# Retention attention and two expert layers on one core: one causal mask for all steps, loads in another order, sums moved forward, paired transposes

## The reference

```python
for t in range(S):                       # q, k, v: (4, 8, 768, 64)
    state = gamma * state + k[:, :, t]^T v[:, :, t]
    y[:, :, t] = scale * q[:, :, t] @ state
x = y as (3072, 512)
h = x @ w_in                             # 512 x 2048
x = where(h > 0, h, exp(min(h, 0)) - 1) @ w_out
h = x @ w_in2                            # 512 x 1024
sm = exp(h - max) / (sum + 1e-9);  s = h * sm
out = ((s - mean(s)) / sqrt(var(s) + 1e-6) * g_ln) @ w_out2
```

## Time and profile before

| | us |
|---|---|
| median of 3 runs (lowest to highest) | 857.64 (855.99 to 858.91) |
| the profiled execution, as timed | 856.04 |
| its span | 854.3 |
| PE busy / DVE / ACT / POOL | 840.5 / 553.7 / 419.0 / 390.1 |
| attention stage, to the first product of the first expert stage | 86.3 |
| first expert stage | 86.3 to about 580 |
| second expert stage and its output | about 580 to 854 |

### The profile page before, as it was taken

How to read it: one execution, slowest core, us unless ns; L and a number is a source line. 1 busy time by engine, 2 the same in 40 slices (tenths; PEclk the granted TensorE clock), 3 DMA queues, 4 the chain that set the end, 5 groups by cost and what they waited for, 6 DMA issues and landing times.

```text
span 854.3 us, 12592 instructions
## 1 busy us (share of the span) xinstructions
PE 840.5 (98%) x4852; PEld 694.9 (81%) x4852; DVE 553.7 (65%) x848; ACT 419.0 (49%) x679; POOL 390.1 (46%) x446
## 2 busy tenths in 40 slices
PE   9997999999999999999999999999999999999998
PEld 6987788888888888888888888887878888888886
DVE  3585667677735455576345655788887777777773
ACT  4566665655525555544355565563333333333322
POOL 3577667575006657540256651464253343444200
PEclk9999999999999999999999999999999999999999
DMA  8999611013103001050111101613011111111001
GB/s 305 362 369 347 228 30 45 25 50 128 49 1 96 28 25 49 26 173 1 43 56 31 44 26 44 203 50 98 26 50 50 49 49 39 51 50 50 25 13 50
DMA packets 49359, 73.32 MB, mean 86 GB/s; under 512 B 3218, under 2 KB 23954, under 8 KB 49044
## 3 DMA queue, kind: packets, MB, share of 16 engines
q1 hardware_dynamic: 48864, 72.43, 25.2%
q10 hardware_dynamic: 436, 0.08, 0.0%
HBM read 55.73 MB, written 16.78 MB: 85 GB/s over the span
## 4 chain that ended last, share of the span: by engine, by line
PE 92%; DVE 4%; ACT 1%; issue 1%; POOL 1%; DVEq 0%; ACTq 0%; POOLq 0%
PE ps L673 10%; PE ps L677 10%; PE ps L674 10%; PE ps L626 9%; PE ps L628 9%; PE ps L627 9%; PE ps L783 5%; PE ps L785 5%; PE ps L784 5%; PE ps L685 4%; PE ps L687 4%; PE ps L686 4%; PE ps L576 3%; PE ps L603 3%; PE ps L769 2%; PE ps L589 1%
## 5 line engine op out<-in xcount | busy, mean ns | idle before, releaser
L494 POOL TENSOR_TENSOR u_lo<-u_raw,u_hi 128x256 fp32r<-128x256 f32 x168 | 142.0, 878 | 193.5 <-ACT u_hi L1117 193.5
L673 PE MATMUL ps<-g_hi,wd_hi 128*128 128x512 f32 x384 | 149.4, 389 | 0.0
L674 PE MATMUL ps<-g_hi,wd_lo 128*128 128x512 f32 x384 | 149.4, 389 | 0.0
L677 PE MATMUL ps<-g_lo,wd_hi 128*128 128x512 f32 x384 | 149.4, 389 | 0.0
L626 PE MATMUL ps<-x_hi,u_hi 128*128 128x512 f32 x336 | 131.3, 391 | 1.2 <-DVE u L888 1.2
L627 PE MATMUL ps<-x_hi,u_lo 128*128 128x512 f32 x336 | 130.8, 389 | 0.0
L628 PE MATMUL ps<-x_lo,u_hi 128*128 128x512 f32 x336 | 130.7, 389 | 0.0
L489 POOL TENSOR_TENSOR u_raw<-u_raw 128x256 f32<-128x256 f32 x96 | 88.7, 923 | 17.3 <-DMA u_raw<-w_dram 11.1
L677 PEld LDWEIGHTS ps<-g_lo,wd_hi 128*128 128x128 f32 x384 | 72.1, 188 | 15.0
L674 PEld LDWEIGHTS ps<-g_hi,wd_lo 128*128 128x128 f32 x384 | 72.1, 188 | 15.0
L673 PEld LDWEIGHTS ps<-g_hi,wd_hi 128*128 128x128 f32 x384 | 72.1, 188 | 14.9
(11 more groups left out here) (91 smaller groups left out, 1498.1 us busy)
## 6 DMA issues: line engine op xcount, KB each, us to landing
u_raw<-w_dram SPq DMA_DIRECT2D x24, 512.0 KB, 3.5
k<-units_dram SPq DMA_DIRECT2D x12, 512.0 KB, 6.4
q<-units_dram SPq DMA_DIRECT2D x12, 512.0 KB, 4.8
v<-units_dram SPq DMA_DIRECT2D x12, 512.0 KB, 7.3
x_between<-x SPq DMA_DIRECT2D x24, 256.0 KB, 2.7
x_raw<-x_between SPq DMA_DIRECT2D x12, 512.0 KB, 3.5
out_dram<-y_sb SPq DMA_DIRECT2D x24, 256.0 KB, 2.0
kn<-units_dram SPq DMA_DIRECT2D x10, 512.0 KB, 6.1
```

What stands on the lines that cost most here:

```text
L494: nc.gpsimd.tensor_tensor(u_lo[n % 2][:, o, :], u_raw[n % 2][:, o, :], u_hi[n % 2][:, o, :].bitcast(f32), ALU.subtract).then_inc(ul_done, 1)
L673: nc.tensor.matmul(ps[:, bank + m, :], hi, g_hi[:, no % 3, :], start=(f == 0), stop=False)
L674: nc.tensor.matmul(ps[:, bank + m, :], lo, g_hi[:, no % 3, :], start=False, stop=False)
L677: last = nc.tensor.matmul(ps[:, bank + m, :], hi, g_lo[:, no % 3, :], start=False, stop=(f == NF1 - 1))
```

## The change

It has five parts.

1. The table `mask0`, the two-row table and the three `spread_row` products go. A full-size `q_decay` table (256 KB) is loaded by SP first; DVE scales q of step 0, and POOL scales q of every later step, step 6 among them. All steps use the same causal mask. PE's warm-up products go from 6 to 13.
2. `load_step(s)` issues q(s), v(s), k(s) and natural k(s), all of the same step.
3. In the first expert stage, unit 0 does U3 ahead of the activation and the weight split, and unit 1's U2 is done ahead of the last activation of unit 0.
4. In the second expert stage DVE's sums for products 1 and 2 are done earlier, the moments being cut in two (`solu_spread`, `solu_variance`); in the last pair the second maximum is taken after the first tile's variance.
5. From the third pair on (`separate` is false) P7 comes before P5, P5 and P3 use bank 4 in place of bank 6, and both tiles of a pair are transposed one after the other, the odd one into banks 6 and 7.

```diff
-WARM = 6
+WARM = 13
...
+        def separate(u):
+            return u < 3
+        def P5(u):
+            return 4 if separate(u) else 5
+        def P7(u):
+            return 5 if separate(u) else 4
+        def w_bank(u):
+            return 6 if separate(u) else 4
+        def normed_bank(t):
+            return 0 if t < 4 else 6 * (t % 2)
...
-                step_over(s - SLOTS)
-                load(s, v_sb, 3, v_in)
-                if s + 1 < NS:
-                    step_over(s + 1 - SLOTS)
-                    load(s + 1, q_sb, 0, q_in)
+                if s >= SLOTS:
+                    sp.wait_ge(att_done, s - SLOTS + 1)
+                load(s, q_sb, 0, q_in)
+                load(s, v_sb, 3, v_in)
+                load(s, k_sb, 1, k_in)
                 if s % NC < NC - 1:
                     load(s, kn_sb, 2, kn_in)
-                if s + 1 < NS:
-                    load(s + 1, k_sb, 1, k_in)
...
-            load(0, k_sb, 1, k_in)
-            load(0, q_sb, 0, q_in)
+            sp.dma_start(q_decay[:, :], tables[:, T_QDEC:T_QDEC + HH * C]).then_inc(q_decay_in, 16)
...
-                if (s + 1) % NC > 0:
+                if s + 1 < NS:
                     decay_q(s + 1)
...
-                if u > 0:
-                    pe.wait_ge(h2_summed, sums(u - 1, H12))
-                up_product(u, W, S1, T1, True)
+                if separate(u):
+                    if u > 0:
+                        pe.wait_ge(h2_summed, sums(u - 1, H12))
+                    up_product(u, ps[:, w_bank(u), :], S1, T1, True)
                 pe.wait_ge(h2_summed, sums(u, U2))
                 up_product(u, Y, S3, T3, False)
+                if not separate(u):
+                    pe.wait_ge(h2_copied, u + 1)
+                    up_product(u, ps[:, w_bank(u), :], S1, T1, True)
...
-            pe.wait_ge(rows_in, 16)
-            spread_row(0, 4)
-            spread_row(1, 5)
...
                 norm_transposes(t)
+                if not separate(p):
+                    norm_transposes(t + 1)
                 last_products(p + 1)
...
+            dve.wait_ge(q_decay_in, 16)
+            dve.wait_ge(q_in[0], 16)
+            for one in range(2):
+                nc.vector.tensor_tensor(q_sb[0][:, one, :], q_sb[0][:, one, :], q_decay[:, :], ALU.mult)\
+                    .then_inc(q0_decayed, 1)
...
-                keep_sum(u2[:, :], n, U2, h21, Y, M6)
-                activate(e11, n, G11, X)
-                if blk == 0:
-                    wd_split_lo(2 * i)
+                if n != 1:
+                    keep_u2(n)
+                if n > 0:
+                    activate(e11, n, G11, X)
+                    if blk == 0:
+                        wd_split_lo(2 * i)
                 keep_sum(u3[:, :], n, U3, h21, Y, M7)
+                if n == 0:
+                    activate(e11, n, G11, X)
+                    wd_split_lo(0)
...
                 split_g_lo(down_no(blk, 0, 2 * i + 1), e21)
+                if n == 0:
+                    keep_u2(1)
                 activate(stash[:, 2 * i, :], n, G12, stash[:, 2 * i, :])
...
-                solu_max(t + 3)
+                if not final:
+                    solu_max(t + 3)
                 solu_product(t + 2)
-                solu_moments(t + 2)
+                solu_spread(t + 2)
+                solu_variance(t + 2)
+                if final:
+                    solu_max(t + 3)
                 solu_normalise(t + 2)
...
-                solu_moments(t + 3)
+                solu_spread(t + 3)
                 if p == 0:
-                    add(u3[:, :], 2, U3, kept, Y, P7)
+                    add(u3[:, :], 2, U3, kept, Y, P7(2))
+                solu_variance(t + 3)
```

More of the change, by code:

```diff
@@ L48, with build @@
 TILE_OF = {place_of(n): n for n in range(NCH)}
-def build(nc, units, w1, w_in2, w_out2, g_ln, tables, rows_table, x_dram, x2_dram, out):
+def build(nc, units, w1, w_in2, w_out2, g_ln, tables, x_dram, x2_dram, out):
     f32, f32r = mybir.dt.float32, mybir.dt.float32r
@@ L563, in scores @@
                 pe.wait_ge(k_in[slot], 16 * loads(s))
[L564 to L567, removed]
+                if s > 0:
+                    pe.wait_ge(q_decayed, s)
                 for one in range(2):
-                    if s > 0:
+                    if s == 0:
+                        pe.wait_ge(q0_decayed, one + 1)
+                    else:
                         pe.wait_ge(masked, 2 * s - 1 + one)
@@ L764, in norm_transposes @@
                 pe.wait_ge(soft[t % 2], SOFT * (t // 2 + 1))
-                pe.wait_ge(nl_done, 2 * t)
+                if t == 5:
+                    pe.wait_ge(h2_summed, sums(2, H12))
+                else:
+                    pe.wait_ge(nl_done, 2 * t if t <= 4 else 2 * (t - 1))
                 for q in range(2):
@@ L863, in split_x_lo @@
                 nc.vector.tensor_tensor(x_lo[:, o], x_raw[:, o], x_hi[:, o].bitcast(f32), ALU.subtract).then_inc(xl_done, 1)
-            for s in range(NS):
[L866 to L874, removed]
+            dve.wait_ge(q_decay_in, 16)
[3 more added lines that the diff above has]
+                    .then_inc(q0_decayed, 1)
+            dve.wait_ge(causal_in, 16)
+            for s in range(NS):
                 apply_mask(s, 0)
@@ L977, in last_sums @@
                 add(h2[:, 1, 0:512], u, H21, kept, Y, P4)
-                add(h2[:, 0, 512:1024], u, H12, u2[:, :], W, P3)
+                add(h2[:, 0, 512:1024], u, H12, u2[:, :], ps[:, w_bank(u), :], P3)
             def normalised_lo(t):
@@ L1134, in _ @@
             decay_v(0)
-            act.wait_ge(spread, 3)
-            nc.scalar.activation(q_decay[:, :], ps[:, 7, :], ACT.Copy).then_inc(q_decay_made, 1)
             for s in range(NS):
@@ L1250, in normalised_hi @@
                     part = slice(q * (NF2 // 2), (q + 1) * (NF2 // 2))
-                    nc.scalar.activation(n_hi[:, t % 2, part, :], ps[:, q, :].rearrange("p (f t) -> p f t", t=P), ACT.Copy)\
+                    nc.scalar.activation(n_hi[:, t % 2, part, :], ps[:, normed_bank(t) + q, :].rearrange("p (f t) -> p f t", t=P), ACT.Copy)\
                         .then_inc(nh_done, 1)
@@ L1319, in decay_tables @@
     state_decay = np.tile(gamma[head] ** C, (1, 2))
-    q_rows = (scale * gamma[:, None] ** (t + 1)[None, :]).reshape(2, HH * C)
-    first, second = np.eye(2)
-    both = np.arange(P) // D == np.arange(2)[:, None]
-    rows = [q_rows, np.tile(first[:, None], (1, P)), np.tile(second[:, None], (1, P)), both]
-    return (np.concatenate([causal, np.eye(P), v_decay, state_decay], axis=1).astype(np.float32),
-            np.concatenate(rows, axis=1).astype(np.float32))
+    q_decay = scale * gamma[head][:, :, None] ** (t + 1)[None, None, :]
+    parts = [q_decay.reshape(P, HH * C), causal, np.eye(P), v_decay, state_decay]
+    return np.concatenate(parts, axis=1).astype(np.float32)
 def kernel(q, k, v, moe_w_in, moe_w_out, moe2_w_in, moe2_w_out, moe2_g_ln):
```

90 lines of the change are left out of this document (43 added, 47 removed).

## The result

The changed kernel takes 848.03 us (median of 7 runs, 847.68 to 849.79) against 855.99 us for the kernel before on the same chip: a ratio of 0.9913, 95% interval 0.9891 to 0.9934. The forecast was 855.9 with a range down to 850.5, so the gain was about 8 us where 1.75 was expected. The profiled spans are 846.1 and 854.3.

What follows compares the result with a forecast made beforehand. PE, with 92% of the chain of waits, was taken to bound the kernel. Attention -2.4, units -0.5, opening -0.25, pairs +0.9 and last pair +0.5 gave -1.75 us, so 855.9 against 857.64, range 850.5 to 860.5.

Steps and rivals of the forecast that it cites:

- The failed step: Attention, step 8: PE's instruction fetch waits behind all loads queued by then, starts at 59.5, pause ends at 61.8.
- The forecast's count of the queue: Attention: 12.5 load units, then 29 of 512 KB (15.2 MB), stand ahead of the instruction fetch.
- The first rival: Attention: loads keep up, the fetch isn't held back, PE alone sets the pace; attention -6.5, kernel 851.8; chance 26%.
- The start: Step 0 of attention: scores start near 8.7, step 1 between 14.4 and about 17, taken as 16, against 17.98.
- The wait for y: Attention at 69.74: PE's 1.29 us wait for ACT to evacuate y of step 8 goes, as v loads second.
- Units 0 and 1: First expert stage: loss at U3(0) goes, new wait of about 1.1 us behind ACT's copy; -0.5 us, bounds -1.5 to 0.
- The opening: Second expert stage's start: waits for U2 and U3 go, those for normalised tiles come next; -0.25 us, between -1.3 and +0.3.
- The pairs: Second expert stage, third pair on: new 0.87 us wait at P7 of product 3; sum +0.9 us, between -0.15 and +2.
- The 0.15 of the next pair: One pair after product 3: P7 wants 661.8 but U2 ends at 661.9, a wait of 0.15 us.
- The other term: Pairs: one 0.02 us cost of changing from transposes to products goes in each pair, 0.15 us less in all.
- The last pair: Second expert stage's end: sum H12 0.83 us later, second maximum behind the variance; transposes +0.5 us, between -0.5 and +1.3.

Runs made afterwards that it cites:

- four waits removed: Changed kernel with four small edits (W's own bank for product 3, earlier ACT copy in unit 1, DVE order in the opening and last pair): 845.44 us, ratio 0.9902.
- no pairing: Changed kernel with W always in its own bank, a pair's two transposes always apart and P5 ahead of P7: 847.85 us, ratio 0.9928.

## Why the prediction was wrong

- **The failed step** is "is served when the loads queued by then are through". From it followed a pause at 61.8 in step 8, which held attention to 83.6. The changed kernel has no pause in steps 8 to 11: the fetch starts 2.5 to 3.1 us behind the crossing with 2.9 MB or more queued. The forecast's count of the queue was right: 41.5 units were out when PE crossed at 50.74, and they were through at 58.45 (forecast 59.5). But the fetch had begun at 53.27, 5.2 us ahead of that. The trace of the kernel before could have told: the rule fits its block 8, and is 2.1 and 2.0 us off at the other two (queue through at 60.47 and 66.98, fetches at 58.34 and 64.99). Nor do its pauses grow with the queue, as was held against the rival: 0.52, 0.66 and 1.88 us stand at 2.30, 2.54 and 2.45 MB. The first rival (loads keep up, 26%) had this right; it gave attention an end near 79 and the kernel 851.8, itself 3.8 us too high: 1.65 by the baseline (see below), the rest mostly by the start. The Trainium skill's rule that the prediction set beside it (DMA: Bandwidth & Descriptors, section Queues, rings and completion order: an engine takes turns between queues at each packet) is nearer to the trace than my queue was, but not the whole of it: by it alone block 8 of the kernel before would not start 6.7 to 7.2 us late.
- **The start.** Scores of step 0 at 9.14 (forecast 8.7; its own terms, 9.75 less half a load of 1.3, give 9.1), step 1 at 14.44, the early end of the forecast 14.4 to 17; I took 16. The condition for it was named: PE at full speed. The kernel before starts step 1 at 17.98 in one profile and 16.00 in the other, so about 2 us of the difference of 8.6 in attention is that one profile's slow step 0.
- **The wait for y** (1.29) going because v is the second load: right, and larger than I made it. It is the one wait that every kernel with v last or third shows (1.49, 1.46, 1.33, 0.95, 0.77).
- **Units 0 and 1**, forecast -0.5, measured -0.49, with the new wait behind ACT's copy that was named. ACT, then PE, of the changed kernel:

```profile
93.36 0.58 ACT L1204 ACTIVATE p<-ps 128x512 f32<-128x512 f32 x1
```

```profile
93.99 0.50 PE L627 MATMUL ps<-x_hi,u_hi 128*128 128x512 f32 x1 [0.83 <-ACT p L1204]
```

- **The opening**, forecast -0.25, measured +0.38. The waits for U2 and U3 went as said, but T(0) waits 1.42 us and T(3) 1.29: with U2 ahead of the moments, DVE has nothing to do for the 0.67 us in which POOL makes the power of the column, which U2 had filled before. PE's timeline:

```profile
587.15 1.06 PE L770 MATMUL ps<-ident,e 128*128 128x128 f32 x8 [1.42 <-DVE e L1046]
...
614.83 0.84 PE L770 MATMUL ps<-ident,e 128*128 128x128 f32 x6 [1.29 <-DVE n_lo L997]
...
631.61 0.50 PE L686 MATMUL ps<-x_hi,u_hi 128*128 128x512 f32 x1 [0.72 <-DVE u L976]
```

- **The pairs**, forecast +0.9. The wait at P7 of product 3 is the last row above: the spacing there is 1.11 us instead of 0.23, 0.88 lost, 0.87 forecast. The 0.15 of the next pair did not come. The other term was mis-sized: a period has gone from 22.40 to 22.31 us, 0.6 over seven of them, where I had 0.15.
- **The last pair**: DVE is idle 1.31 us for the exponential and takes the second maximum afterwards, as forecast; T(22) comes 0.15 us later, not 0.5. DVE's timeline:

```profile
821.11 1.23 DVE L1015 TENSOR_TENSOR e<-e,h 128x1024 f32<-128x1024 f32 x1 [1.31 <-ACT e L1268]
...
824.26 1.21 DVE L1008 TENSOR_REDUCE stats<-h 128x1 f32<-128x1024 f32 x1
```

Outside attention the sum of the forecast was +0.65 and the measurement +0.49; that is luck, since the opening missed by 0.6 one way and the two terms of the pairs by 0.6 and 0.35 the other. In attention it was -2.4 against -8.6 between the two profiles, and -6.1 against the second profile of the kernel before. The forecast also counted from the shown median, 857.64; later runs of the kernel before had medians of 854.35 to 855.99, so part of the distance to 848.03 is that baseline.

## What to carry to other kernels

A transfer's place in its batch is priced by the engine that has to work on it first, and by what stands behind that work in the engine's program: here v had to be early for ScalarE, since the copy that PE waited for came after it. When a wait's cause is inferred from a single place (a fetch that came late behind a queue), test it on the other blocks of the same trace before it is carried over to a new order; here two of three didn't fit. And take a second profile of the kernel before, if it can be had: between two of them step 1 began at 17.98 and at 16.00, and two of the three pauses were gone.

## What the runs showed of the hardware

- In attention PE paused at the start of a block of instructions only where it came there early: it went on 1.3 to 1.6 us after the end of the block's fetch (0.9 us long). Not each arrival as early as that paused (1.37 and 1.48 without a pause); none with 1.8 us or more did.
- SyncE's issue of a load takes 0.47 us, but 1.63 in the changed kernel where an instruction fetch starts just then (45.34), and 1.33 and 1.38 in the kernel before, where fetches start at 58.34 and 64.99:

```profile
44.77 0.47 SPq L338 DMA_DIRECT2D k<-units_dram  x1
45.28 1.63 SPq L338 DMA_DIRECT2D kn<-units_dram  x1
```

- In step 0 the 32 score products took 3.79 us in both profiles of the kernel before and 2.06 in the changed one, with a granted clock of 1.00 shown in all three. So the clock of the record does not tell here at which speed they ran. Where the start is the changed kernel's, they took 2.06 us in two executions (the changed kernel, four waits removed) and 3.05 in a third (no pairing); the granted clock in 10 to 12 was 1.00 in the first two and 0.52, the 1.2 GHz level, in the third, and attention ended 0.9 to 1.0 us later there. With 13 warm-ups and another load order they took up to 3.46 us.
